# Two-layer FFN behind a pooled attention: the last product's weights 192 bytes on, one sum and two roundings in other places

## What is computed

```python
attn = softmax(q @ mean8(k).T / sqrt(64)) @ mean8(v)   # 8 batches, 8 heads, 576 queries, 72 pooled keys
x = attn.transpose(0, 2, 1, 3).reshape(4608, 512)
h = x @ w1_in;  g = max(0.01 * h, h);           x = g @ w1_out    # 512 -> 2048 -> 512
h = x @ w2_in;  g = h * clip(h + 3, 0, 6) / 6;  out = g @ w2_out  # 512 -> 2048 -> 512
```

## The kernel before

| matmuls | weights | moving operand | weights minus moving |
|---|---|---|---|
| first products, layer 1 | ring: 128 | xs_hi, xs_lo: 64 | 64 |
| second products, layer 1 | wout: 128 | g_hi, g_lo: 64 | 64 |
| first products, layer 2 (`STREAM_AT` = 16 words on) | ring: 192 | xs_hi, xs_lo: 128 | 64 |
| second products, layer 2 (`SECOND_AT` = 32 words on) | g_hi, g_lo, gs: 192 | wout, w_sums: 128 | 64 |

## Time and profile before

### The profile page before, as it was taken

The page is one execution under the profiler, slowest core; times in us unless marked ns, Lnnn a source line. Parts: engine busy times, 40 slices in busy tenths (PEclk is TensorE's granted clock), DMA queues, the critical chain, the costliest instruction groups (busy, mean ns, idle before and its releaser), DMA issues. The chain is left out here.

```text
span 1664.3 us, 40092 instructions
## 1 busy us (share of the span) xinstructions
PE 1650.5 (99%) x13914; PEld 1627.9 (98%) x13914; DVE 1126.6 (68%) x2159; ACT 676.8 (41%) x1427; POOL 433.5 (26%) x451
## 2 busy tenths in 40 slices
PE   9999999999999999999999999999999999999998
PEld 8999999999999999999999999999999999999998
DVE  6768777686776867755555666676767676766665
ACT  5554443243333333333323544444444444344433
POOL 4346552021211212112426562111111111111100
PEclk9999999999999999999999999999999999999999
DMA  7746878678686786858779998898989898989884
GB/s 235 256 144 220 281 250 264 224 232 263 199 267 212 238 256 205 279 178 281 237 262 354 318 327 309 298 334 285 331 283 330 294 330 281 336 294 334 283 310 153
DMA packets 228572, 447.94 MB, mean 269 GB/s; under 512 B 23872, under 2 KB 48448, under 8 KB 219200
## 3 DMA queue, kind: packets, MB, share of 16 engines
q1 hardware_dynamic: 228416, 445.74, 79.9%
HBM read 379.58 MB, written 66.06 MB: 268 GB/s over the span
## 5 line engine op out<-in xcount | busy, mean ns | idle before, releaser
L1781 PE MATMUL ps_h<-xs_hi,ring 128*128 128x256 f32 x3808 | 805.4, 282 | 4.5 <-DVE h L1447 3.0
L1781 PEld LDWEIGHTS ps_h<-xs_hi,ring 128*128 128x128 f32 x3808 | 639.3, 189 | 10.6 <-issue 7.0
L1781 PE MATMUL ps_h<-xs_lo,ring 128*128 128x256 f32 x1904 | 531.3, 279 | 0.0
L1781 PEld LDWEIGHTS ps_h<-xs_lo,ring 128*128 128x128 f32 x1904 | 359.0, 189 | 0.0
L1129 ACT ACTIVATE g_hi<-gate 128x512 fp32r<-128x512 f32 x288 | 182.0, 632 | 380.1 <-DVE gate L1381 194.3
L1727 PE MATMUL ps_y<-g_hi,wout_hi 128*128 128x256 f32 x1152 | 320.7, 278 | 0.6 <-DVE y_stage L1443 0.6
L1727 PE MATMUL ps_y<-g_hi,wout_lo 128*128 128x256 f32 x1152 | 319.9, 278 | 0.0
L1727 PE MATMUL ps_y<-g_lo,wout_hi 128*128 128x256 f32 x1152 | 319.8, 278 | 0.0
L1727 PEld LDWEIGHTS ps_y<-g_hi,wout_hi 128*128 128x128 f32 x1152 | 216.7, 188 | 0.9 <-DVE y_stage L1443 0.8
L1727 PEld LDWEIGHTS ps_y<-g_lo,wout_hi 128*128 128x128 f32 x1152 | 217.2, 189 | 0.0
L1727 PEld LDWEIGHTS ps_y<-g_hi,wout_lo 128*128 128x128 f32 x1152 | 216.3, 188 | 0.0
(11 more groups left out here) (153 smaller groups left out, 2862.8 us busy)
## 6 DMA issues: line engine op xcount, KB each, us to landing
ring<-w_in_split SPq DMA_DIRECT2D x920, 256.0 KB, 4.0
w_sums<-w_out_sums SPq DMA_DIRECT2D x64, 1024.0 KB, 6.2
w_in_split<-ring SPq DMA_DIRECT2D x56, 256.0 KB, 3.7
w_in_split<-stage SPq DMA_DIRECT2D x56, 256.0 KB, 4.0
k_raw<-in_kT SPq DMA_DIRECT2D x32, 288.0 KB, 4.4
q_raw<-in_qT SPq DMA_DIRECT2D x32, 288.0 KB, 5.1
v_raw<-in_v SPq DMA_DIRECT2D x32, 288.0 KB
x0T<-x_stage SPq DMA_DIRECT2D x32, 288.0 KB, 4.2
```

What stands on the lines that cost most here:

```text
L1781: mm = pe.matmul(banks[BANK_OF[r]], a, b[:, r, c, :], start=r in OPENS and c == 0 and n == 0, stop=c == 1 and n == 2, skip_group_check=True)
```

## The change

Three edits.

1. Slot 6 of each ring, the weights of a step's last product, starts 48 words (192 bytes) further on, in both layers (`LAST_AT`). Its weights then start at 64 modulo 256 in layer 1 and at 128 in layer 2, where the moving operand of that product starts at 64 and 128: weights minus moving is 0 for these six matmuls. The rings had these bytes to spare.
2. `t_sums` is split. `t_first` makes T1, and waits for the upper rows' two loads alone (`x_loaded` is now a pair of semaphores). `t_rest` makes the other three and waits for the lower rows' loads. In the loop over tiles `t_first` stands ahead of the last `v_lo` of attention. ACT's rounding of B11 waits for the upper loads alone.
3. In tiles 7 to 16 ACT rounds only blocks 0 to 4 of the next tile at step 7. NT4 is rounded at step 0 of the tile itself behind `p1`, B22 behind the copy of h's first quarter. DVE's lower parts follow: NT4 behind step 0's lower gate, B22 behind the add of h's lower right quarter.

```diff
-LATE_X_HI_AT = (0, 1, 2, 3, 4, 5)
+LATE_X_HI_AT = (0, 1, 2, 3, 4)
+LAST_AT = 48
...
         def ring_slot(q, second=False):
-            return ring[q % RING // PRODUCTS][second][:, q % PRODUCTS]
+            r = q % PRODUCTS
+            at = r * 4 * P + STREAM_AT * second + (LAST_AT if r == PRODUCTS - 1 else 0)
+            return ring[q % RING // PRODUCTS][:, at:at + 4 * P].rearrange("p (a f) -> p a f", a=4)
...
-                             ).then_inc(x_loaded, 16)
+                             ).then_inc(x_loaded[c // 2], 16)
...
-            def t_sums(T, attention=True):
-                pool.wait_ge(x_loaded, 64 * T)
+            def t_first(T, attention=True):
+                pool.wait_ge(x_loaded[0], 32 * T)
                 if attention:
                     above_zero(pool, x_ready, PRODUCTS * (T - 1))
                 else:
                     wait_x(pool, T - 1)
+                nc.gpsimd.tensor_tensor(t_sum[:, SUM_AT[T1]], x_stage[:, 0:2, HN:N],
+                                        x_stage[:, 0:2, 0:HN], ALU.subtract
+                                        ).then_inc(t_summed, 1)
+            def t_rest(T):
+                pool.wait_ge(x_loaded[1], 32 * T)
                 t1, t2, t3, nt4 = [t_sum[:, SUM_AT[r]] for r in (T1, T2, T3, NT4)]
-                nc.gpsimd.tensor_tensor(t1, b12, b11, ALU.subtract).then_inc(t_summed, 1)
                 pool.wait_ge(t_summed, 4 * T - 3)
...
+                stores2_done(i + 1)
+                t_first(T + 1)
                 if next_unit:
                     v_lo(T + 2, 0)
-                stores2_done(i + 1)
-                t_sums(T + 1)
+                t_rest(T + 1)
...
-                    x_hi(T, B22, layer == 2)
+                    x_hi(T, NT4, layer == 2)
                 g_hi_of(s - 1, (i - 1) % HF, 0, before if i == 0 else layer)
...
                 nc.scalar.activation(h[:, 0, 0:HN], banks[0], ACT.Copy).then_inc(c11_ready, 1)
+                if i == 0 and last_x and not attention:
+                    x_hi(T, B22, layer == 2)
...
                 gate_of(s - 1, 0, last)
                 if i == 0 and not attention and not ends_x:
-                    x_end_lo(T, B22)
+                    x_end_lo(T, NT4)
...
                 add(h[:, 1, HN:N], 0, u3[:]).then_inc(c22_ready, 1)
+                if i == 0 and not attention and not ends_x:
+                    x_end_lo(T, B22)
...
-                if i == HF - 1 and not attention and next_end:
-                    x_end_lo(T + 1, NT4)
```

More of the change, by code:

```diff
@@ L217, in ffn_attention_kernel @@
         for c, groups in ((1, (0, 2)), (2, (1, 3))):
-            slots = sb(f"ring{c}", [P, PRODUCTS * 4 * P + 64], F32R)
-            ring.append([slots[:, at:at + PRODUCTS * 4 * P].rearrange(
-                "p (r a f) -> p r a f", r=PRODUCTS, a=4) for at in (0, STREAM_AT)])
+            ring.append(sb(f"ring{c}", [P, PRODUCTS * 4 * P + 64], F32R))
             units[c] = overlaid(lambda sb: attention_buffers(sb, c, 4096))
@@ L365, in ffn_attention_kernel @@
         ring_loaded = [sem(f"ring_loaded{i}") for i in range(RING)]
-        x_loaded = sem("x_loaded")
+        x_loaded = [sem(f"x_loaded{i}") for i in range(2)]
         t_summed = sem("t_summed")
@@ L892, in t_sums @@
                     wait_x(pool, T - 1)
-                b11, b21, b12, b22 = [x_stage[:, 2 * j:2 * j + 2, n * HN:(n + 1) * HN]
-                                      for n in range(2) for j in range(2)]
+                nc.gpsimd.tensor_tensor(t_sum[:, SUM_AT[T1]], x_stage[:, 0:2, HN:N],
[3 more added lines that the diff above has]
+                pool.wait_ge(x_loaded[1], 32 * T)
+                b12, b21, b22 = x_stage[:, 0:2, HN:N], x_stage[:, 2:4, 0:HN], x_stage[:, 2:4, HN:N]
                 t1, t2, t3, nt4 = [t_sum[:, SUM_AT[r]] for r in (T1, T2, T3, NT4)]
-                nc.gpsimd.tensor_tensor(t1, b12, b11, ALU.subtract).then_inc(t_summed, 1)
                 pool.wait_ge(t_summed, 4 * T - 3)
@@ L913, in split_x @@
             def split_x(T):
-                t_sums(T, attention=False)
+                t_first(T, attention=False)
+                t_rest(T)
                 x_lo(T)
@@ L992, in _ @@
             v_lo(2, 0)
-            t_sums(1)
+            t_first(1)
+            t_rest(1)
             pool.wait_ge(x_ready, 4)
@@ L1000, in _ @@
                     v_lo(2, {2: 1, 4: 2, 5: 3}[i])
-            t_sums(2)
+                if i == 5:
+                    t_first(2)
+            t_rest(2)
             v_lo(3, 0)
@@ L1095, in x_hi @@
                     act.wait_ge(t_summed, 4 * (T - 1) + (T1, T2, T3, NT4).index(r) + 1)
-                elif r == B11:
-                    act.wait_ge(x_loaded, 64 * T)
+                elif r in (B11, B21):
+                    act.wait_ge(x_loaded[r == B21], 32 * T)
                 nc.scalar.activation(xs_hi[second][:, r], x_block(r), ACT.Copy
@@ L1602, in step @@
             def step(T, i, layer, before=None, attention=False, ends_x=False, piece_at=(),
-                     first_piece=0, next_unit=True, pairs=False, next_end=True):
+                     first_piece=0, next_unit=True, pairs=False):
                 s = HF * T + i
@@ L1704, in _ @@
             for i in range(HF):
-                step(ALL_TILES - 1, i, 2, pairs=True, next_end=False)
+                step(ALL_TILES - 1, i, 2, pairs=True)
             s = HF * ALL_TILES - 1
```

## The result

| | before | after |
|---|---|---|
| median of the runs (lowest, highest), us | 1667.27 (1663.10, 1670.92), 5 runs | 1678.54 (1677.46, 1679.54), 5 runs |
| the profiled execution, us | 1666.07 | 1678.83 |
| its span, us | 1664.3 | 1677.0 |

The changed kernel is slower: ratio 1.0068, 95% interval 1.0045 to 1.0091. The forecast was 1644 us. Lines have moved in the changed kernel: the first products are line 1796 (1781 before), the second ones 1742 and 1883 (1727, 1868), DVE's adds 1462 (1447), the gate 1402 (1387), POOL's sums 896 to 909.

A forecast was written before the change was run, and what follows sets the result against it. PE was taken as the bound, through its waits and two matmul spacings. Terms -19.3 - 4.1 - 1.5 = -25 us from 1666.1 gave 1641; with half the median's 4.7 us excess kept, 1644 us, range 1636 to 1652.

The forecast's parts named there:

- What bounds the kernel: Whole kernel: PE busy 1650.5 of 1664.3 us; only its waits and its two matmul spacings, 4.3 ns apart, can move time.
- the long spacing of tiles 7 to 17: Layer-2 matmuls starting 0.1176 instead of 0.1134 us apart; claimed to cost 22 us, all of it to be gained.
- Edit 1: Product 6, tiles 1 to 17: shifted weights pass every step to the short spacing; -19.3 us, between -25 and a loss.
- the crossing: Start of tile 9, PE going from layer 2's product to layer 1's: one weight load at the moving row's residue.
- The reading of tile 9: At its start, all 8 crossings without a wait came from the long spacing, and the short one appeared behind them.
- what six in a row cost: Product 6's six matmuls at difference 0: taken as 0.03 us a step over 136 steps, 4 us, between 0 and 6.
- Edit 2: Starts of tiles 2 to 7: T1 made early removes PE's gaps; -4.1 us, between -2 and -4.1.
- Edit 3: Step 0 of tiles 10 to 17: later NT4 and B22 rounding removes product 2's gap; -1.5 us, at worst 0.
- Rival B: Product 6: difference 0 is the bad case and hands on the long spacing; slower, 1696 us; chance 0.15.
- the collisions: Product 6 under Rival B: six matmuls in a row collide where the crossing had one; plus 6 us.
- The excess of the median over the profiled execution: Kernel before: median 4.7 us above the profiled execution, taken as spacing too, half of it to stay.
- Rival A: Product 6: addresses set no spacing, or difference 0 flips it either way; 1653 to 1675 us, middle 1662; chance 0.28.

The follow-up runs named there:

- the table: Ten placements of product 6's weights and x, each in the changed kernel with its two other edits kept; medians from 1644.84 to 1678.54 us.

## Why the prediction was wrong

**What bounds the kernel: right.** PE's two spacings, and that they are inherited until something disturbs them, is what the whole result turns on. The forecast priced the long spacing of tiles 7 to 17 at 22 us; the excess in the trace is 20.8 + 1.5 = 22.3. Weights on by 128 bytes took 18.2 + 1.3 us of it away.

**Edit 1: the failed step.** It is the sentence "If it acts like the crossing, every step passes to the short rhythm at its end and holds it until the next disturbance." The reading of tile 9 was right as far as it went: one load at difference 0 turns the long spacing short, and the kernel with both operands on by 192 bytes does just that inside product 6 in the steps that arrive long (median distances 121, 121, 116, 114, 114 ns). The step from one load to six was not in the trace. With six, the distances are 120 ns and the long spacing is left behind, from either state. Six in a row isn't the whole of it either: with x moved instead, five loads at difference 0 inside product 6 and one on the way out leave the short spacing. What failed is the choice of the difference at one crossing as the thing that decides. The working said itself that "what six in a row cost isn't in the trace", but took that as a question of price (0 to 6 us; it was 3.3 - 1.5 + 1.5 - 0.1 = 3.2) and not of sign. The term was -19.3 us; the spacing in product 6 and around it measured +16.5 in the trace (10.2 + 1.8 + 3.1 + 1.4), and between the medians with and without the shift lie 14.3 us (1678.54 and 1664.29).

**Edit 2: the removed gaps right, the net too large.** The gaps at the tile starts cost before (4247 - 6 * 117 + 6 * 75) ns = 4.0 us by the distances, and all but some 0.4 went in the kernel with this edit alone. What the step left out is the layer-2 tiles: there too all of POOL's sums come earlier, and a gate falls on one of them. The forecast did write that "should it slow DVE at a bad moment it costs some 0.1 us in each of five tiles"; it cost 0.3 to 0.8 in each of six, 2.0 us net of what before had. -4.1 + 0.4 + 2.0 is -1.7; measured were -3.0 us (0.9982), between -6.3 and +0.3, so no effect of this edit on the time is shown for sure.

**Edit 3: right in the trace, too small to be timed.** All eight gaps are gone, 8 * 0.18 us by the same count as in the forecast. The measured ratio was 0.9999, from -3 to +3 us. In step 2 of tiles 13 and 16 a gap of 0.35 us stands ahead of product 4, about 0.6 us together; the kernel with the 128 bytes alone has one of these too (tile 16), so it needn't come from this edit.

**Rival B was the case, its size was not.** It put the point of decision where it was: "the matmuls behind product 6 are at 117.6 ns". It had 0.15. Its +25 us was 14 too much: tiles 1 to 6 lost 3.1 us rather than 12, since there the long spacing that product 6 leaves doesn't last through a step (the mean distance inside product 0 rose from 115.7 to 117.6 ns, inside product 1 only from 114.8 to 115.5), with attention's matmuls in between; the collisions cost 3.2 rather than 6; tiles 7 to 17 lost 10.2 of the 13 it gave them.

**The excess of the median over the profiled execution.** The forecast took the 4.7 us for spacing drawn anew in each run. Much supports this. The kernel with the late blocks alone was profiled in an execution of 1656.38 us, 8.8 below its median: there 57 of the 88 steps are short to short, in before's 31. Kernels whose product 6 lets both spacings pass can spread widely (without the shift 1656.79 to 1670.89 over 12 runs), those that force one lie close together in most cases (1644.25 to 1645.28 over 4 runs, the changed kernel 1677.46 to 1679.54 over 5). It isn't so throughout: x alone on by 64 bytes forces short and spreads from 1645.27 to 1653.26, x alone on by 192 bytes lets both pass and spreads from 1658.95 to 1663.44. And in the measurement of the result before's median was 1667.27, only 1.2 us above the profiled execution, so the half of the excess that the forecast let stand, 2.4 us, is within what the median itself moves by.

**Rival A: half right after all.** It held that difference 0 may flip the spacing "either way". In the kernel with both operands on by 192 bytes the same load on the way in turned 83 long ones short and 4 short ones long. The Trainium skill's two independent read ports ("TensorE: Matmul & The Clock Gate", section "Step-by-step: what each phase is for"), by which a weight load takes nothing from the running matmul, have no place for what was measured, and the measurement decides: the same instructions took 1644.84 and 1678.54 us with nothing but 64 bytes between the places of a seventh of the first products' weights.

**What stays open.** Why the spacing has two values and what in the pair of addresses chooses. Neither the difference nor the weights' place orders the table: difference 0 stands in a row that forces long and in one that forces short; weights on by 48 words force long with x at 0 or 48 and turn over with x at 16. The loads on the way in and out count too, as the kernels with both operands moved show, but not by their difference alone: with both on by 192 bytes the way out at difference 128 goes with short turning long in 83 steps, with x alone on by 192 bytes the way out has the same difference and 40 steps stay short. The table is measured at these ten places, in this kernel's order of products, and tells nothing sure about an eleventh. That 256 bytes is the period was taken for granted: no run moved an operand by 256 bytes.

## What to carry to other kernels

When PE is full and at full clock, compare the number of like matmuls in stretches of equal length: if two stretches differ, there may be a second rhythm to be won, and 64 bytes more or less of padding at one operand of one product can win or lose it, as they did here. Try several paddings and count the spacing behind the product for each, instead of deducing the one from a single crossing; a state that is inherited must be tested from both states and with as many loads in a row as the change has. And an engine's work that is moved earlier in one phase of a shared routine is moved earlier in all its phases: look at what it will run beside there.

## What the runs showed of the hardware

- Float32 matmuls of 128 by 256 behind one another, each with its weight load, start 113.3 or 117.8 ns apart at the same full clock, for over 400 in a row, and 120 ns apart in product 6 of the changed kernel.
- The spacing is a state: ten placements of one product's operands gave four behaviours, forcing short, forcing long, holding what comes, and turning it over at each step.
- A gate of DVE that began together with POOL's sum took 1.84 us instead of 0.71, and POOL's sum its usual 1.29.
- In two of the profiled executions the granted clock fell for a stretch of tile 0 to the lower level, with matmuls 213 ns apart, after PE had waited 1.3 us; in others a wait of 1.2 us at the same place left it full.
